# A different opening for each iteration of a kernel that interleaves attention with two feed-forward networks

## The reference

```python
kv_flat = kv_pool.reshape(B, -1, C) @ w_sr          # 768 keys, k = v = kv_flat
s = scale * (q @ k.transpose(0, 2, 1))
a = np.exp(s - s.max(-1, keepdims=True))
a /= a.sum(-1, keepdims=True) + 1e-09
x = a @ v
h = x @ w_in1;  x = (h * sigmoid(1.702 * h)) @ w_out1            # first network
h = x @ w_in2;  out = (h * np.clip(h + 3, 0, 6) / 6) @ w_out2    # second network
```

## Time and profile before

| | us |
|---|---|
| time, median of 3 runs | 1321.69 (1320.3 to 1322.43) |
| time of the profiled execution | 1322.82 |
| its span, first to last instruction | 1321.1 |
| PE busy in the span | 1282.8 (97%) |
| DVE busy | 1042.9 (79%) |
| ACT busy | 1034.2 (78%) |

### The profile page before, as it was taken

The page is one execution under the profiler, slowest core; times in us unless marked ns, Lnnn a source line. Parts: engine busy times, 40 slices in busy tenths (PEclk is TensorE's granted clock), DMA queues, the critical chain, the costliest instruction groups (busy, mean ns, idle before and its releaser), DMA issues.

```text
span 1321.1 us, 18302 instructions
## 1 busy us (share of the span) xinstructions
PE 1282.8 (97%) x5748; PEld 1061.3 (80%) x5748; DVE 1042.9 (79%) x1073; ACT 1034.2 (78%) x1211; POOL 36.1 (3%) x43
## 2 busy tenths in 40 slices
PE   6789999999999999999999999999999999999996
PEld 6578888888888888888888888888888888888775
DVE  4778788788888888788888887888888788788666
ACT  2678778788788787887877878878878778788665
POOL 1900000000000000000000000000000000000000
PEclk9999999999999999999999999999999999999999
DMA  8322213113022032130230321312303213112000
GB/s 263 93 62 63 54 19 72 37 35 72 11 61 63 8 72 46 25 72 20 52 70 1 72 48 24 72 29 43 72 2 69 54 17 72 38 26 65 8 0 17
DMA packets 186948, 65.94 MB, mean 50 GB/s; under 512 B 108720, under 2 KB 179504, under 8 KB 186672
## 3 DMA queue, kind: packets, MB, share of 16 engines
q1 hardware_dynamic: 186928, 65.69, 22.1%
HBM read 23.13 MB, written 6.34 MB: 22 GB/s over the span
## 4 chain that ended last, share of the span: by engine, by line
PE 84%; DVE 7%; ACT 5%; issue 2%; DMA 1%; DVEq 0%; ACTq 0%; SPq 0%
PE pair L784 13%; PE pair L786 13%; PE pair L785 13%; PE bank_av L784 8%; PE bank_av L786 8%; PE bank_av L785 8%; PE bank_out L784 7%; PE bank_out L786 6%; PE bank_out L785 6%; DVE mid_lo L662 3%; DVE work L655 3%; ACT mid_hi L459 2%; ACT work L446 2%; PE pair L798 1%; DMA kv_sb<-in_kv_dram 1%
## 5 line engine op out<-in xcount | busy, mean ns | idle before, releaser
L662 DVE TENSOR_TENSOR mid_lo<-work,mid_hi 128x1024 fp32r<-128x1024 f32 (+1 forms) x193 | 235.2, 1219 | 117.9 <-ACT mid_hi L459 117.6
L784 PE MATMUL pair<-x_hi,w_hi 128*128 128x512 f32 x768 | 302.2, 394 | 6.6 <-DVE x_lo L638 5.5
L785 PE MATMUL pair<-x_lo,w_hi 128*128 128x512 f32 x768 | 299.6, 390 | 0.0
L786 PE MATMUL pair<-x_hi,w_lo 128*128 128x512 f32 x768 | 299.5, 390 | 0.0
L646 DVE TENSOR_TENSOR mid_lo<-work,mid_hi 128x1024 fp32r<-128x1024 f32 x192 | 237.4, 1237 | 53.9 <-ACT mid_hi L438 53.9
L431 ACT ACTIVATE work<-pair 128x1024 f32<-128x1024 f32 x192 | 196.9, 1026 | 105.8 <-PE pair L786 105.7
L655 DVE SCALAR_TENSOR_TENSOR work<-work,pair 128x1024 f32<-128x1024 f32 (+1 forms) x193 | 233.1, 1208 | 8.5 <-ACT work L446 8.4
L459 ACT ACTIVATE mid_hi<-work 128x1024 fp32r<-128x1024 f32 (+1 forms) x193 | 202.3, 1049 | 29.5 <-DVE work L655 28.1
L446 ACT ACTIVATE work<-pair,half 128x1024 f32<-128x1024 f32 (+1 forms) x193 | 211.5, 1097 | 11.1 <-PE pair L786 10.4
L438 ACT ACTIVATE mid_hi<-work 128x1024 fp32r<-128x1024 f32 x192 | 202.0, 1052 | 4.9 <-PE bank_av L786 3.4
L784 PEld LDWEIGHTS pair<-x_hi,w_hi 128*128 128x128 f32 x768 | 144.5, 188 | 44.6 <-DVE x_lo L638 6.3
(11 more groups left out here) (87 smaller groups left out, 1506.9 us busy)
## 6 DMA issues: line engine op xcount, KB each, us to landing
p_keys<-p_turned SPq DMA_DIRECT2D x368, 96.0 KB, 2.2
inv_b<-inv_dram SPq DMA_DIRECT2D x24, 256.0 KB, 3.2
q_raw<-in_q_dram SPq DMA_DIRECT2D x92, 64.0 KB, 2.0
out_dram<-y_sb SPq DMA_DIRECT2D x92, 64.0 KB, 2.4
kv_sb<-in_kv_dram SPq DMA_DIRECT2D x7, 768.0 KB, 11.7
w_raw<-in_moe_w_in_dram SPq DMA_DIRECT2D x2, 1024.0 KB, 8.5
inv_dram<-inv_t SPq DMA_DIRECT2D x96, 0.5 KB
kv_sb<-in_kv_dram SPq DMA_DIRECT2D x3, 256.0 KB, 11.7
```

The costliest lines, as they stand in the source:

```text
L662: dve.tensor_tensor(mid_lo[mid2(t, p)][:, part], act2[p % 2][:, part], mid_hi[mid2(t, p)][:, part], ALU.subtract).then_inc(mid2_ready, 1)
L784: pe.matmul(dst, a_hi, b_hi, start=start, stop=False)
L785: pe.matmul(dst, a_hi, b_lo, start=False, stop=False)
L786: return pe.matmul(dst, a_lo, b_hi, start=False, stop=stop)
```

## The change

On PE an iteration now opens with h2(0), then h1(0), then P2(7) of the iteration before, which used to close that iteration; h1(1), h2(1), P1(0), h1(2), P2(0) follow as they did. Iteration 1 has no such P2(7), and the last one's stands behind the loop. ACT opens with gate(0), then gelu(0), act1_hi(0), act2_hi(0), gelu(1), act1_hi(1), gate(1). DVE opens with `turn_p` of slots 1 and 2, then hard_swish(0), `turn_p` of slot 3, act1_lo(0), act2_lo(0), `turn_y`, and then act1_lo(1). The instructions are the same ones and as many; from pair 2 on the order is as it was.

```diff
 def iteration(i, ...):                       # ACT
     for p in range(PAIRS):
+        if p == 0:
+            gate(i - 1, p)
+        if p == 1:
+            act2_hi(i - 1, p - 1)
         gelu(i, p)
+        if 1 < p < PAIRS - 1:
+            act2_hi(i - 1, p - 1)
+        act1_hi(i, p)
         if p == PAIRS - 1:
-            act1_hi(i, p)
             act2_hi(i - 1, p - 1)
-        else:
-            if p > 0:
-                act2_hi(i - 1, p - 1)
-            act1_hi(i, p)
-        gate(i - 1, p)
+        if p > 0:
+            gate(i - 1, p)
...
 def iteration(i, ...):                       # DVE
     for p in range(PAIRS):
-        if p > 0:
-            hard_swish(i - 1, p - 1)
-        if p == 1 and with_p:
-            turn_p(i + 1, 3)
-        if p == 0 and with_y:
-            turn_y(i - 2)
         if p == 0 and with_p:
             turn_p(i + 1, 1)
             turn_p(i + 1, 2)
+        if p == 0:
+            hard_swish(i - 1, p)
+        if p == 0 and with_p:
+            turn_p(i + 1, 3)
+        if p > 1:
+            hard_swish(i - 1, p - 1)
...
-        if 0 < p < PAIRS - 1:
+        if 1 < p < PAIRS - 1:
             act2_lo(i - 1, p - 1)
         act1_lo(i, p)
+        if p == 0:
+            act2_lo(i - 1, p)
+            if with_y:
+                turn_y(i - 2)
...
 def iteration(i, ...):                       # PE
-    for j in range(JOBS):
+    job(i, 1)
+    job(i, 0)
+    if later(i - 1):
+        finish_job(i - 1, JOBS - 1)
+    for j in range(2, JOBS):
         job(i, j)
...
     finish_job(i, JOBS - 3)
-    finish_job(i, JOBS - 1)
...
 iteration(NT - 1, scored_too=False, weighed=False)
+finish_job(NT - 1, JOBS - 1)
```

## The result

The changed kernel takes **1311.86 us** (median of 6 runs, 1310.43 to 1314.29), the kernel before, run beside it on the same chip, 1322.32 us. The ratio is **0.9928, 95% interval 0.9918 to 0.9938**: faster by 9.5 us on 1322.32 (the two medians alone are 10.5 us apart). The forecast was 1315.0 us, 6.7 us faster, with a range down to 1312.8.

The account below looks back on a forecast made before the run. PE bounds the kernel, busy 1282.8 of 1321.1 us. Twenty turns winning 0.37 - 0.07 = 0.30 us each give 6.0, with the written-out iterations 6.7: 1321.7 - 6.7 = 1315.0 us, range 1312.8 to 1319.3.

Parts of the forecast that it names:

- two long steps: PE, each loop opening: steps too long by 0.10 us at h1(1) and 0.37 us at P2(0); the rest plain.
- h1(1)'s 0.10 us: PE's wait at h1(1) for gelu(0), expected to stay, since gelu(0) still starts at 669.00.
- Rival B: ACT's loop opening: gate(0) starts late behind the jump and delays gelu(0); slower, up to 1333.6 us; chance 0.06.
- The new wait at P1(0): PE, loop opening: act1_lo(0) comes late, so P1(0)'s second matmul starts at 673.25 instead of 673.18, 0.07 us a turn.
- The sum for DVE: Seven DVE operations without a pause, from x_lo at 666.36 to the end of act1_lo(0) at 672.86.
- lower bound: No wait at P1(0) if DVE's turns follow as closely as the best pair; 8.5 us won at most.
- P2(0)'s wait: PE, loop opening: 0.37 us a turn behind late act2_lo(0), expected to go with the earlier gate(0) and hard_swish(0).
- The written-out iterations: Three iterations outside the loop's 20 turns: the last wins 0.37 us, the other two 0.15 each.
- fixed base: Median of the kernel before, 1321.7 us, from which the forecast gain of 6.7 us was subtracted.
- A: DVE's row ahead of P1(0) is 0.25 us later, the wait 0.32; 1.7 us left, 1320.0 us; chance 0.13.
- C: P2(0) still waits, for the turn of y, or h2(0) waits for the exponential; nothing won, 1321.7; chance 0.05.
- D: No wait at P1(0), and part of h1(1)'s 0.10 us goes too; 9.0 us won, 1312.7; chance 0.04.

Follow-up runs that it names:

- e4_slot3_behind: Changed kernel with DVE's turn of slot 3 moved behind act2_lo(0) and the turn of y; 1312.57 us, ratio 0.9934 to the kernel before.
- e1_after_again: Changed kernel run once more, unaltered; 1311.58 us, ratio 0.9930 to the kernel before.
- g1_swap_two: Changed kernel with h2(1) ahead of h1(1), P2(0) ahead of h1(2), gate(1) ahead of gelu(1), slot 3's turn behind the turn of y; 1311.96 us, ratio 0.9924.
- g4_both: g1_swap_two with the turn of y right behind hard_swish(0) and gelu(0) freed of its second wait; 1307.50 us, ratio 0.9897 to the kernel before.
- e5_gelu_one_wait: Changed kernel with slot 3's turn moved as in e4_slot3_behind and gelu(0) freed of its second semaphore wait; 1308.41 us, ratio 0.9902 to the kernel before.
- e2_pe_alone: Kernel before with only PE's new order, plus DVE's turn of y behind the turns of slots 1 and 2; 1321.72 us, ratio 0.9999.
- e3_y_turn_ahead: Changed kernel with the turn of y put ahead of act1_lo(0) on DVE; 1325.50 us, ratio 1.0029 to the kernel before.
- e5b_gelu_again: Same kernel as e5_gelu_one_wait, run again; 1310.64 us, ratio 0.9916 to the kernel before.
- f0_before_fill: Kernel before with 14 matmuls belonging to no result in PE's hole ahead of the first h1(0); 1320.16 us, ratio 0.9990.

## Why the prediction was right in its direction and short in its size

**What bounds the kernel: right.** PE does, and only its two long steps were worth something. (The scores' matmuls, of 384 columns, step by 0.17 us and not by the plain 0.227, against the forecast's reading of the rest of the iteration; nothing hangs on it.) The long step at P2(0) went in every turn, and with it 18.9 - 6.8 = 12.1 us of weight-loader wait.

**PE's and ACT's steps: right.** h2(0) and P2(7) met nothing late. gate(0) came right behind the warming activation and gelu(0) stayed 0.12 us behind h1(0), so h1(1)'s 0.10 us stayed. Rival B, by which the first work behind the loop's jump is late, is refuted by gate(0)'s 0.11 us behind the start of the warming activation; the branch rule of the Trainium skill (Runtime: NRT & Kernel Launch, Instruction fetch mechanics) did not show here in either order. No run shows whether the jump's target lay outside the fetched window, so the rule itself was not tested.

**The new wait at P1(0): the step that failed.** The forecast put 0.07 us there, at the second matmul; it measured 0.01 at that matmul, and 0.04 with the slow steps behind it (e4_slot3_behind). The sum for DVE came out 0.10 us too long: 0.05 from the length of act1_lo(0), 1.18 where the forecast took the 1.23 of the earlier trace rows, 0.03 from the step behind hard_swish(0), 1.10 instead of 1.13, and 0.01 each at two turns. In the loop's opening of before no such operation stood right behind a transpose: each had idle time or another tensor operation ahead of it. In the new order both do, and there they are shorter. The forecast had named this as its lower bound ("nothing, if DVE's turns follow each other as closely as the best pair shows") and then took the middle. The price of P2(0)'s wait was short by the same kind of slow steps: behind its 0.37 us stand six steps that the forecast took for plain ("within a hundredth"), 0.025 us together. Counted alike, P2(0)'s wait was 0.40 us a turn and P1(0)'s is 0.04, which leaves 0.36; a turn got 0.354 shorter, where the forecast had 0.30. Over the 20 turns that is 7.09 - 6.0 = 1.1 us too little, some 0.6 of it from P1(0) and 0.5 from P2(0). That DVE's row is what decides, with no slack, was right: 0.60 us more cost 0.58.

**The written-out iterations: nearly right.** 0.67 us forecast; 0.14 + 0.29 + 0.45 = 0.88 measured.

**The sum and the range: a term put at nothing.** 7.97 us in the traces, 1321.7 - 8.0 = 1313.7 on the forecast's own base, would lie inside the range. So the mis-sized wait alone did not take the median out of it; what did is the opening, whose change from run to run the forecast put at nothing when it took 1321.7 for a fixed base. The measured difference, 9.5 us by the ratio and 10.5 by the medians, holds 1.5 to 2.5 us more than the turns and the written-out iterations give, and by elimination those lie ahead of the second x_hi: behind it the profiled executions without a fall of the clock there are 8.0 to 8.4 us apart (1232.1 to 1232.4 against 1224.0 to 1224.1), and with the hole of the opening filled the medians themselves are 8.06 apart.

In that stretch executions of the same code differ by 2 us, by where the clock's fall lands. All fourteen profiled executions sort by it. In the eight with a long iteration 0 (38.3 to 38.9 us) h1(0) ran at the lower level almost from its start; in the six with a short one (36.3 to 36.9) at least its first three matmuls ran at the full one. A fall behind these cost iteration 0 nothing: 36.80 us in e1_after_again and 36.29 in g1_swap_two, against 36.82 in g4_both and 36.30 in e5_gelu_one_wait without a fall. The start of iteration 0 differs by up to 1.8 us besides (first x_hi at 48.5 to 50.2 us). The range held only errors of the sum; the three times of before, 1320.3 to 1322.43, already showed a scatter of 2 us that it should have taken in.

Whether the changed kernel meets the short opening more often than the kernel before, which its medians suggest, and by what, stays open: its mean granted clock per run (0.997 or 0.998) does not tell the forms apart, since the kernel before took 1319.5 us and 1322.6 us at 0.998. An estimate from the medians (less 1.7 us, by which time and span differ in the profiled executions, less the stretch behind) puts the second x_hi at 86.0 and 85.8 us in the two rounds of the changed kernel and at 87.1 to 88.5 in four of the kernel before, but at 87.7 to 88.2 for e2_pe_alone, e3_y_turn_ahead, e4_slot3_behind and e5b_gelu_again, which have the changed kernel's order on PE too. So the short opening does not come with that order every time; nothing in the forecast pointed to it, and that the gain came out larger for it was, as far as the forecast goes, chance.

**The rivals.** A and C did not come: P1(0) is 0.04 us late in the mean and P2(0) on time. D, with 1312.7 nearest to the result, was right in its first half (hardly a wait at P1(0)) and wrong in its second (h1(1)'s wait stayed whole).

## What to carry to other kernels

When a moved operation lands within 0.1 us of the slot of the engine that bounds the kernel, its row has to be summed with spacings that were read behind the same kind of neighbour; where the trace has none, both ends of the bound belong into the forecast with equal right. A wait's price does not end with its long step: the slightly slow steps behind it belong to it, up to the next plain one. Before a scatter between runs is taken for noise around the forecast, cut the span at a recurring mark: here what lies behind the second x_hi repeated to 0.4 us in the three kernels that were profiled twice, and most of the scatter lay in an opening of 89 us. The cut does not catch all of it: in f0_before_fill a fall of the clock behind the mark cost 1.2 us. And a wait that is removed shows the next one at once: P2(0), then h1(1), then the turn of y, each worth 0.1 to 0.4 us a turn, and each found in the same 15 us of the timeline.

## What the runs showed of the hardware that was not expected

- A DVE operation of 128x1024 right behind a transpose lasted 1.18 us, and the next started 1.10 us later; behind another tensor operation or an idle stretch 1.21 to 1.23 us, with 1.13 to 1.14. These are medians over all fourteen traces, 525 operations behind a transpose and over 8000 others. It shows in the changed kernel for hard_swish(0) and act1_lo(0), and in e3_y_turn_ahead for act1_lo(0) behind the turn of y (1.18).
- An activation that waits for its semaphore itself (gelu(0) in e5_gelu_one_wait) started 0.03 to 0.04 us behind the matmul that released it, one with a register instruction ahead of it that waits, 0.12 us.
- Behind a matmul held up by a late operand (P2(0) in the kernel before) the second one started 0.34 us later instead of 0.23, and the six steps after it were 0.001 to 0.006 us too long, 0.025 together. P1(0) in the changed kernel, hardly late, had 0.24 us and then 0.024 in nine steps.
- PE's clock fell to its lower level at the idle stretch of 2.8 to 3.3 us ahead of the first h1(0), or soon behind it, in ten of the twelve executions that have this stretch; in the other two (e5_gelu_one_wait, 2.8 us, and g4_both, 3.3 us) it did not fall there at all. In the kernel before with this hole filled it fell behind one of 2.2 us in iteration 1; in the two profiled executions of the kernel before without the filling, which have the same 2.2 us there, it did not.
